# Attention on one core: the division by the softmax sums moved behind the product with the values, and that product done in runs

## The reference

```
scores = scale * np.matmul(q, k.transpose(0, 1, 3, 2))
scores = scores + bias.transpose(2, 0, 1)[None, :, :, :]
scores = scores - np.max(scores, axis=-1, keepdims=True)
attn = np.exp(scores)
attn = attn / (np.sum(attn, axis=-1, keepdims=True) + 1e-09)
return np.matmul(attn, v).astype(np.float32)
```

## Time and profile before

| | |
|---|---|
| median of three runs | 1266.7 us (1266.56 to 1267.24) |
| span of the profiled execution, first to last instruction | 1264.6 us |
| its own time beside the span | not given apart; the median lies 2.1 us above the span |
| bias phase | to about 67 us |
| attention | 67 to 364 us |
| the two layers | from 364 us |
| TensorE busy in the span | 1219.2 us |
| mean granted TensorE clock | 0.995 of full speed |

### The profile page before, as it was taken

The page is one execution under the profiler, slowest core; times in us unless marked ns, Lnnn a source line. Parts: engine busy times, 40 slices in busy tenths (PEclk is TensorE's granted clock), DMA queues, the critical chain, the costliest instruction groups (busy, mean ns, idle before and its releaser), DMA issues. The chain is left out here.

```text
span 1264.6 us, 26124 instructions
## 1 busy us (share of the span) xinstructions
PE 1219.2 (96%) x9106; PEld 1096.9 (87%) x9106; DVE 725.5 (57%) x1764; ACT 526.9 (42%) x1188; POOL 497.8 (39%) x588
## 2 busy tenths in 40 slices
PE   6789999999979999999999999999999999999998
PEld 2266777777669999999999999999999999999998
DVE  8977777777779777878778788552112020211111
ACT  6977777777723434344444433212212121212111
POOL 3056666666666424344243444551111111111111
PEclk9989999999999999999999999999999999999999
DMA  5844425252135000000000002340000000000000
GB/s 183 248 146 136 141 95 160 92 179 66 64 95 147 2 1 0 0 0 1 0 0 0 0 0 67 92 117 20 1 19 19 0 19 0 19 0 19 0 19 19
DMA packets 47590, 69.06 MB, mean 55 GB/s; under 512 B 3744, under 2 KB 28480, under 8 KB 47552
## 3 DMA queue, kind: packets, MB, share of 16 engines
q1 hardware_dynamic: 47552, 68.60, 17.4%
HBM read 53.25 MB, written 15.34 MB: 54 GB/s over the span
## 5 line engine op out<-in xcount | busy, mean ns | idle before, releaser
L817 PE MATMUL banks<-x_high,w_high_rest 128*128 128x288 f32 x992 | 293.3, 296 | 0.5 <-PEq L1010 0.5
L818 PE MATMUL banks<-x_low,w_high_rest 128*128 128x288 f32 x992 | 292.8, 295 | 0.0
L819 PE MATMUL banks<-x_high,w_low_rest 128*128 128x288 f32 x992 | 291.8, 294 | 0.0
L1372 DVE TENSOR_TENSOR product<-angle_or_silu,banks 128x288 f32<-128x288 f32 x96 | 43.4, 452 | 312.2 <-PE banks L819 312.2
L1391 POOL TENSOR_TENSOR product_low<-product,product_high 128x288 fp32r<-128x288 f32 x96 | 77.6, 808 | 356.4 <-ACT product_high L1332 356.4
L1190 POOL TENSOR_TENSOR product_low<-product,product_high 128x288 fp32r<-128x288 f32 x128 | 110.4, 863 | 242.5 <-ACT product_high L1070 242.5
L817 PE MATMUL bank<-product_high,w_high_rest 128*128 128x288 f32 x672 | 201.3, 300 | 3.5 <-POOL product_low L1391 2.0
L819 PE MATMUL bank<-product_high,w_low_rest 128*128 128x288 f32 x672 | 197.8, 294 | 0.0
L818 PE MATMUL bank<-product_low,w_high_rest 128*128 128x288 f32 x672 | 197.7, 294 | 0.0
L819 PEld LDWEIGHTS banks<-x_high,w_low_rest 128*128 128x128 f32 x992 | 186.7, 188 | 0.0
L817 PEld LDWEIGHTS banks<-x_high,w_high_rest 128*128 128x128 f32 x992 | 185.9, 187 | 0.7 <-issue 0.7
(11 more groups left out here) (97 smaller groups left out, 2539.4 us busy)
## 6 DMA issues: line engine op xcount, KB each, us to landing
raw_qk<-in_qk SPq DMA_DIRECT2D x32, 576.0 KB, 3.7
bias_scratch<-bias_stage SPq DMA_DIRECT2D x36, 288.0 KB, 3.1
bias<-bias_scratch SPq DMA_DIRECT2D x32, 288.0 KB, 3.1
w_raw<-in_w_out SPq DMA_DIRECT2D x28, 256.0 KB, 2.6
values<-in_v SPq DMA_DIRECT2D x16, 320.0 KB, 4.0
w_raw<-in_w_in SPq DMA_DIRECT2D x16, 256.0 KB, 2.9
out_t<-X SPq DMA_DIRECT2D x7, 576.0 KB, 3.0
w_raw<-in_w_gate SPq DMA_DIRECT2D x12, 256.0 KB, 3.0
```

Of the source, the lines that this page charges most:

```text
L817: nc.tensor.matmul(out, high, x_high, start=start, stop=False)
L818: nc.tensor.matmul(out, high, x_low, start=False, stop=False)
L819: return nc.tensor.matmul(out, low, x_high, start=False, stop=stop)
L1372: dve.tensor_tensor(s[:, :], silu[:, :], val_ps[f % 2][:, 0:NT], ALU.mult).then_inc(s_ready, 1)
```

## The change

The probabilities are no longer normalised. The transposes wait for the exponentials alone, and `T_LAG` falls from 4 to 3. The sums of a head's five tiles are guarded in one instruction and inverted in one, VectorE's `reciprocal` with the five columns read 64 times each, so that `inv_total` holds 128 x 5 x 64 values a head. TensorE transposes these (`spread`, five transposes a pair, in slots 3 and 4, into free columns of the score banks), VectorE copies them to `inv_spread`, and `divide` multiplies the product by them as it leaves its bank, where `keep_mixed` copied it before. The product is now in two parts of 256 and 320 queries, each in two runs: blocks 0 and 1 in slots 4 and 7, blocks 2, 3 and 4 in slots 5 and 8 of the next pair. VectorE copies the transposed tiles 2 and 7, ScalarE the other eight. GpSimd prepares queries and keys only, and afterwards splits all eight first weights in a row. The end of the last pair is written out anew.

```
-EXP_LAG, T_LAG = 2, 4
+T_LAG = 3
...
-    total = sb(ctx, "total", [P, TILES], F32)
-    guarded = sb(ctx, "guarded", [P, TILES], F32)
-    inv_total = sb(ctx, "inv_total", [P, TILES], F32)
+    total = sb(ctx, "total", [P, 2, NQ], F32)
+    guarded = sb(ctx, "guarded", [P, 2, NQ], F32)
+    inv_total = sb(ctx, "inv_total", [P, NQ, 2, D], F32)
+    inv_spread = sb(ctx, "inv_spread", [P, S], F32)
...
+    DVE_KEEPS = (2, 7)
+    ACT_KEEPS = [s for s in range(TILES) if s not in DVE_KEEPS]
+
+    PARTS = ((0, 1), (2, 3, 4))
+    MIX_SLOTS = {4: (0, (0, 1)), 5: (0, (2, 3, 4)), 7: (1, (0, 1)), 8: (1, (2, 3, 4))}
+    SPREAD_SLOTS, DIVIDE_SLOTS = {3: 0, 4: 1}, {6: 0, 9: 1}
+
+    def queries_of(part):
+        return slice(PARTS[part][0] * P, min((PARTS[part][-1] + 1) * P, S))
...
+            pool.memset(total[:, :, :], 1.0).then_inc(total_filled, 1)
+            prepare(1, 0)
+            with pool.Fori(1, LAST) as n:
+                prepare(n, 1)
+                prepare(n + 1, 0)
+            prepare(LAST, 1)
+            for w in range(HEAD):
                 weights.split_high(pool, w)
                 weights.split_low(pool, w)
...
+            def spread(n, s, part):
...
+                if part == 0:
+                    pe.wait_ge(inverted, (n + 1) * 2)
+                for i, qt in enumerate(PARTS[part]):
+                    rows, at = rows_of(qt), HS + i // 2 * P
+                    last = nc.tensor.transpose(scores[s % 2][:, i % 2, at:at + rows],
+                                               inv_total[0:rows, qt, :, :].rearrange("p h d -> p (h d)"),
+                                               ident[0:rows, 0:rows])
+                last.then_inc(spread_ready, 1)
...
-                pe.wait_ge(*normed_of(n, s))
+                pe.wait_ge(exped, n * TILES + (s + 1))
                 if not (first and s < 2):
-                    pe.wait_ge(copied, n * TILES + (s - 1))
+                    pe.wait_ge(*(copied_of(n, s - 2) if s >= 2 else copied_of(n - 1, TILES + s - 2)))
...
+                    if not (first and part == 0):
+                        pe.wait_ge(mixed_copied, n * 2 + part)
+                for c in blocks:
+                    if c < NQ - 1:
+                        for h in range(2):
+                            nc.tensor.matmul(mixed[h * D:(h + 1) * D, 0:wide], values[parity][:, c, h, :],
+                                             probs_t[parity][:, h, c, queries], start=(c == 0), stop=False)
+                    else:
+                        pe.wait_ge(end_copied, n + 1)
+                        nc.tensor.matmul(mixed[:, 0:wide], values[parity][:, c, :, :].rearrange("p h d -> p (h d)"),
+                                         probs_t_end[parity][:, queries], start=False, stop=True).then_inc(mixed_ready, 1)
+
+            def slot(n, parity, s, step):
+
+                score(n, s, step == 0)
+                if step > 0 and s in SPREAD_SLOTS:
+                    spread(n - 1, s, SPREAD_SLOTS[s])
+                if s >= T_LAG:
                     turn(n, s - T_LAG, step == 0)
                 elif step > 0:
-                    half, c = divmod(s - 3, NQ)
-                    mix(n - 1, 1 - parity, half, c, step == 1)
+                    turn(n - 1, TILES - T_LAG + s, step == 1)
+                if step > 0 and s in MIX_SLOTS:
+                    mix(n - 1, 1 - parity, *MIX_SLOTS[s], step == 1)
...
-            for s in range(TILES):
-                slot(PAIRS, 0, s, 2, compute=False)
-
+
+            for s in range(TILES - T_LAG, TILES):
+                turn(LAST, s, False)
             pe.wait_ge(biased, PAIRS * TILES)
+            for part in range(2):
+                spread(LAST, part, part)
+            mix(LAST, 1, 0, range(NQ), False)
+            pe.wait_ge(spread_copied, PAIRS * 2)
             chunks.first_h(pe)
-            for c in range(2, NQ):
-                mix(LAST, 1, 1, c, False)
+            mix(LAST, 1, 1, range(NQ), False)
...
+            def guard(n, h):
+
+                dve.wait_ge(exped, n * TILES + (h + 1) * NQ)
+                dve.tensor_scalar(guarded[:, h, :], total[:, h, :], 1e-9, None, ALU.add).then_inc(guard_done, 1)
+
+            def invert(n, h, first):
+                dve.wait_ge(guard_done, n * 2 + (h + 1))
+                if not first:
+                    dve.wait_ge(spread_ready, n * 2)
+                dve.reciprocal(inv_total[:, :, h, :], guarded[:, h, :].unsqueeze(2).broadcast_to([P, NQ, D])
+                               ).then_inc(inverted, 1)
...
+            def keep_spread(n, s, part):
+
+
+                dve.wait_ge(spread_ready, n * 2 + (part + 1))
+                start = PARTS[part][0] * P
+                last = dve.tensor_copy(inv_spread[:, start:start + 2 * P].rearrange("p (a b) -> p a b", a=2),
+                                       scores[s % 2][:, :, HS:HS + P])
+                if part == 1:
+                    rows = S - start - 2 * P
+                    last = dve.tensor_copy(inv_spread[:, start + 2 * P:S], scores[s % 2][:, 0, HS + P:HS + P + rows])
+                last.then_inc(spread_copied, 1)
+
+            def divide(n, part):
+
+                queries = queries_of(part)
+                wide = queries.stop - queries.start
+                dve.wait_ge(mixed_ready, n * 2 + (part + 1))
+                dve.wait_ge(spread_copied, n * 2 + (part + 1))
+                dve.tensor_tensor(X[:, bass.ds(n * S + queries.start, wide)], mixed[:, 0:wide],
+                                  inv_spread[:, queries], ALU.mult).then_inc(mixed_copied, 1)
 
             def pair(n, parity, step, hp=None):
 
                 for s in range(TILES):
...
+                    if step > 0 and s == 2:
+                        guard(n - 1, 1)
+                        invert(n - 1, 1, step == 1)
+                    elif s == 7:
+                        guard(n, 0)
+                        invert(n, 0, step == 0)
+                    if step > 0 and s in SPREAD_SLOTS:
+                        keep_spread(n - 1, s, SPREAD_SLOTS[s])
                     if hp is not None:
                         dve.wait_ge(att.bias_in[s], (hp + 1) * 16)
                     add_bias(n, s, step == 0)
-                    if step > 0 and s == 4:
+                    if step > 0 and s in DIVIDE_SLOTS:
+                        divide(n - 1, DIVIDE_SLOTS[s])
+                    if s - T_LAG in DVE_KEEPS:
+                        keep(n, parity, s - T_LAG)
+                    elif step > 0 and TILES - T_LAG + s in DVE_KEEPS:
+                        keep(n - 1, 1 - parity, TILES - T_LAG + s)
+                    if step > 0 and s == 2:
                         keep_end(n - 1, 1 - parity)
...
+            for s in range(TILES - T_LAG, TILES):
+                if s in DVE_KEEPS:
+                    keep(LAST, 1, s)
+            guard(LAST, 1)
+            invert(LAST, 1, False)
+            for part in range(2):
+                keep_spread(LAST, part, part)
             keep_end(LAST, 1)
-            dve.wait_ge(mixed_copied, (LAST - B + 2) * 2)
             for k in DVE_PARTS:
                 features.high(dve, 0, k)
             for k in range(KC):
                 features.low(dve, 0, 0, k)
-            keep_mixed(LAST, 0)
-            keep_mixed(LAST, 1)
+            divide(LAST, 0)
+            divide(LAST, 1)
```

More of the change, by code:

```diff
@@ L397, in attention_phase, with copied_of, keep_tile @@
     LAST = PAIRS - 1
[L399 to L412, removed]
+    DVE_KEEPS = (2, 7)
[5 more added lines that the diff above has]
+        return slice(PARTS[part][0] * P, min((PARTS[part][-1] + 1) * P, S))
+    def copied_of(n, s):
+        if s in DVE_KEEPS:
+            return dve_copied, n * len(DVE_KEEPS) + (DVE_KEEPS.index(s) + 1)
+        return act_copied, n * len(ACT_KEEPS) + (ACT_KEEPS.index(s) + 1)
+    def keep_tile(eng, n, parity, s):
+        h, qt = s // NQ, s % NQ
+        rows = rows_of(qt)
+        eng.wait_ge(turned_ready, n * TILES + (s + 1))
+        out = probs_t[parity][:, h, :, qt * P:qt * P + rows]
+        turned_in = turned[s % 2][:, 0:(NQ - 1) * rows].rearrange("p (c q) -> p c q", c=NQ - 1)
+        return out, turned_in
     with nc.Block() as block:
@@ L485, in _ @@
[L485 to L493, removed]
         @block.tensor
@@ L533, in turn, with mix @@
                 last.then_inc(turned_ready, 1)
-            def mix(n, parity, half, c, first):
-                if c == 0:
-                    if half == 0:
+            def mix(n, parity, part, blocks, first):
+                queries = queries_of(part)
+                wide = queries.stop - queries.start
+                if 0 in blocks:
+                    if part == 0:
                         pe.wait_ge(att.values_in[parity], n * 8 + (16 - 8 * parity))
-                        pe.wait_ge(copied, n * TILES + (NQ + 3))
+                        pe.wait_ge(*copied_of(n, NQ + 1))
@@ L542, in mix @@
                     else:
-                        pe.wait_ge(copied, (n + 1) * TILES)
```

(22 more changed lines are left out.)

118 lines of the change are left out of this document (30 added, 88 removed).

## The result

The changed kernel took 1304.93 us (median of 4 runs, 1303.41 to 1305.79), the kernel before 1266.97 us beside it. The ratio is 1.0298, with a 95% interval of 1.0284 to 1.0313. "Slower" was the likelier sign (0.62), but 1285 us was 20 us too low and the upper end of the range, 1300, was passed.

What follows compares the result with a forecast made beforehand. TensorE sets attention's pace; a pair goes from 17.70 to 19.3 us, fifteen pairs add 24, the tail gains 5: span 1264.6 to 1283.6, runs 2.1 above, 1285.7, rounded 1285 us. Range 1252 to 1300.

Steps and rivals of the forecast that it cites:

- Slower: Predicted sign for the whole kernel: slower 0.62, same 0.05, faster 0.33.
- guard: VectorE, slot 2: the guard follows slot 1's bias step, from 4.2 to 4.35 us.
- The disputed price: VectorE's 128x320 reciprocal: taken as half fixed, half per element, 2.4 us; case of 1.7 to 3.0 us, chance 0.58.
- R: Time of the wide 128x320 reciprocal on VectorE, taken as 2.4 us.
- rival 1: The wide reciprocal streams, R = 0.4 us; pair 17.55 us, kernel 1257 us; chance 0.32.
- The estimate of 2.7 us: Wide reciprocal at eight cycles an element, 0.96 GHz; pair 0.3 us longer, time near 1289 us.
- What R does in slot 2: R hidden up to 0.9 us; at 2.4 us slot 4's mix starts 1.75 us later, pair 19.3 us.
- The reciprocal of slot 7: Second reciprocal of a pair, under two runs of mix; costs nothing up to R = 3.
- TensorE's own work: TensorE's work for a pair falls from 17.70 to 16.95 us; with 0.6 of stalls the pair takes 17.55.
- switches: TensorE going in and out of lone mix blocks: 0.30 us each, four fewer a pair, 1.20 us saved.
- Pair 0: First pair: earlier transposes gain, the slot-7 reciprocal without mix above it loses; net 0.
- The tail: From last scores to next phase: 20.6 us now, 15.2 in the new order, GpSimd's weights done earlier; gain 5 us.

Runs made afterwards that it cites:

- r9: r4 with no division at all: no widening, spread or spread copies, parts copied out instead of multiplied; 1257.2 us, ratio 0.9929.
- r4: Changed kernel with a 128x5 reciprocal that a VectorE copy widens to 128x320, and without the guard; 1268.2 us, ratio 1.0015.
- r1: Changed kernel without its guard, the addition of 1e-9; the wide reciprocal reads the sums themselves; 1281.0 us, ratio 1.0112.
- r2: Changed kernel with a head's guard as five one-column additions instead of one of 128x5; 1298.3 us, ratio 1.0248.
- r5: Changed kernel with the second head's guard and reciprocal moved from slot 2 to 4, spreads to slots 5 and 6; 1277.1 us, ratio 1.0092.
- r3: Changed kernel with half the reciprocal, 128x160: 32 of 64 copies of each inverse computed, the others stay 1; 1283.3 us, ratio 1.0132.
- r8: Kernel before, division of the probabilities untouched, with only the mix blocks put in runs; 1266.1 us, ratio 0.9994.
- r10: Kernel before, with only two steps at the end of attention reordered, on VectorE and on TensorE; 1261.7 us, ratio 0.9964.

## Why the prediction was wrong, step by step

The runs make a ladder that prices each part of a pair. Each row adds to the one above it:

| part of a pair | forecast, us | measured, us | pair so far, kernel |
|---|---|---|---|
| order of the work, against 17.70 before | -0.70 | -0.14 | 17.56 (r9), 1257.2 |
| spread, widening and multiplication | +0.55 | +0.65 | 18.21 (r4), 1268.2 |
| wide reciprocal (measured: in place of the small one) | +1.75 | +0.69 | 18.90 (r1), 1281.0 |
| guard | 0 | +1.22 | 20.12 (changed), 1304.9 |
| together | +1.60 | +2.42 | |

- **The step that failed: the guard.** "VectorE finishes the bias step of slot 1 at 4.2 and the guard at 4.35": 0.15 us for an instruction that took 1.27. It was priced from the one-column row, though it has five columns and stands beside GpSimd. r1 gives its worth, 24 us of the 38; r2 shows that width matters, r5 that the place does. The trace before held a row of this kind: x_high at 1.62 us for two small casts while GpSimd split weights. I used it for the tail and not for the loop. The loop itself had one as well, VectorE's normalisation, 0.51 us with GpSimd idle and 1.22 us beside its subtraction:

```profile
139.13 0.51 DVE L411 TENSOR_SCALAR probs<-probs,inv_total 128x576 f32<-128x576 f32 x1
...
152.35 1.22 DVE L411 TENSOR_SCALAR probs<-probs,inv_total 128x576 f32<-128x576 f32 x1
```

```profile
151.84 1.42 POOL L350 TENSOR_TENSOR k_low<-raw_qk,k_high 128x576 fp32r<-128x576 f32 x1
```

The rule behind it is in the Trainium skill, "SBUF — State Buffer", section "Who interferes with whom": VectorE shares one pair of ports with GpSimd, copies and `tensor_scalar` between SBUF operands can enter a mode that takes both pairs, and whoever comes second is blocked for the other's whole instruction. The trace agrees in both cases, 1.27 against 0.16 us and 1.25 against 0.36.
- **The disputed price: nearly right.** R was 2.15 us for 2.4, and r3 gives its slope as 6.25 ns an element where I took 7; rival 1, the streaming reciprocal, is out. The estimate of 2.7 us was worked out from the repeat count of 8 in the Trainium skill, "VectorE: DVE Perf Modes", section "First, the fixed hardware budget"; the measured slope is 6 cycles of that page's 0.96 GHz, and the measurement decides.
- **What R does in slot 2: over-priced, and this hid most of the guard's error.** What TensorE waits for is the whole stretch from the end of slot 1's bias step to the inverse. The forecast made it 2.65 us (4.20 to 6.85), hid 1.2 of it and charged 1.75. Measured, the stretch is 1.47 us in r4, 2.15 in r1, 2.44 in r3, 2.57 in r2 and 3.46 in the changed kernel, and the pairs are 18.21, 18.90, 19.13, 19.33 and 20.12: some 1.45 us are hidden, and each us beyond costs a pair one us. r2's stretch is nearly the forecast's and costs 1.12 us over r4. So the lateness of the bias step and of ScalarE's copies behind the reciprocal, which the forecast added on top, was no loss of its own. Reciprocal and guard together cost 1.91 us for the 1.75 forecast. The reciprocal of slot 7 cost nothing, as forecast: slots 7 to 9 take the same 6.6 us in the changed kernel and in r4.
- **TensorE's own work, mis-sized.** The forecast without the spread was 16.95 - 0.55 + 0.6 = 17.0 us; r9 measured 17.56. Its waits for ScalarE are some 0.6 us a pair, as forecast: by the starts, its transposes are 0.43 us late in slot 1, where I had 0.45, and 0.23 in slot 4. So 0.5 us of the 1.20 saved by switches was not there. Some 0.3 of it is the block itself: the earlier trace rows gave 0.131 us a matmul, and in the loop eight of 256 and eight of 320 columns take 1.01 and 1.23 us, 0.14 each, 32 of them in a pair. The last 0.2 was not placed. The spread took 0.92 us of TensorE's time for 0.55, and 0.65 of it reached the pair. This term, 17.55 us forecast for 18.21 with the inverse's wait away, is the second that failed, 0.66 us a pair.
- **The clock, not in the sum.** Three pairs at 21.5 us, 1.35 above the others, are 4 us. In the traces of r1, r3, r4 and r5, where the long wait is short or gone, no pair of the loop fell to the lower clock. That the stall brings the clock down is argued from this order of events; no run held the one and varied the other.
- **Pair 0, costed at nothing.** Its slot 8 took 3.47 us, with TensorE waiting 1.55 for a bias step behind a guard of 1.04 (held again) and a reciprocal of 2.15. The pair went from 13.1 to 15.5 us.
- **The tail: right in kind.** TensorE's and VectorE's timelines of it:

```profile
387.89 0.54 PE L500 MATMUL banks<-k_high,q_parts 128*128 128x288 f32 x1
...
402.07 0.37 PE L846 MATMUL banks<-x_high,w_high_head 128*128 128x288 f32 x1 [0.86 <-PEq L437]
```

```profile
395.18 0.52 DVE L833 CAST x_high<-X 128x288 fp32r<-128x288 f32 x2
395.62 1.56 DVE L840 TENSOR_TENSOR x_low<-X,x_high 128x288 fp32r<-128x288 f32 x4
```

From the last scores to the layer matmul of the earlier trace rows it is 14.2 us for 20.6, a gain of 6.4 where I had 5. The split is 2 us for the 6.1 of the earlier trace rows, since GpSimd is done with its weights, as foreseen.

Two slips changed nothing. The spread copies and divisions on VectorE were priced at 0.34, 0.34, 0.14, 0.34 and 0.41 us, where the rows named for them give 0.43, 0.43, 0.24, 0.43 and 0.49 and the run took 0.42, 0.42, 0.21, 0.42 and 0.48; no term of the sum uses them. And the sum's 1285.7 was written as 1285.

The whole: 14.9 pairs x 2.42 = 36, the clock 4, pair 0 2.4, pair 1 (which had no second half's mix before) 0.9, less 6.4 in the tail, 37 us; the spans differ by 1302.9 - 1264.6 = 38.3. Of the 20 us by which the forecast missed, 12 are the pair (0.82 us, 15 times), 4 the clock and 3 pairs 0 and 1, less 1 in the tail. That r1, without the guard, lands 4 us from the forecast is partly luck: the loop without the wait for the inverse was forecast 0.66 us too short, the wait 1.06 us too dear.

And the gain that could have been had was small from the start. The division's move frees GpSimd, from 146.45 of 215 us to 105.33 of 260, and some of ScalarE, and neither set the end; the runs give TensorE's saving back as waits (r8); only the tail is a gain, and r10 has 4.7 us of it without the change.

## What to carry to other kernels

Price an instruction at its new shape and beside its new neighbours: on VectorE a copy or scalar operation between SBUF operands with more than one element a row can last as long as whatever GpSimd is doing, so look up GpSimd's timeline at each such place, and put the small ones that TensorE waits for where GpSimd is idle. Invert before widening, not after. And in a pipeline whose slots are evenly filled, bunching work to save switches opens the light slots to waits of the same size; test the order alone, with the costly part left out, before tuning the costly part.

## What the runs showed of the hardware

- A reciprocal of float32 on VectorE takes 153 ns and 6.25 ns for each element of a row (128x5 181 ns, 128x160 1153, 128x320 2153). It is not held beside GpSimd: r1's, at 180.15 us with GpSimd's subtraction running since 179.97, takes its usual time (2141 to 2153 ns in all 32), and so does r4's of 128x5 (177 to 189 ns).
- A 128x5 `tensor_scalar` and a 128x320 copy, SBUF to SBUF, were held until GpSimd's `tensor_tensor` ended (1.27 and 1.25 us for 0.16 and 0.36), a 128x576 `tensor_scalar` likewise in the kernel before (1.22 for 0.51); the one-column `tensor_scalar` never was (144 ns in 130 of them).
- Behind a standstill of TensorE of 1.9 to 2.8 us the granted clock was 0.50 to 0.76 of full over the next microseconds (0.69 from 168 to 172 us in the changed kernel, 0.76 and 0.50 from 304 to 308 and 308 to 312 in r2), in some pairs and not in others with the same wait (1.00 from 127 to 131 in the changed kernel).
